# Clustered attention and two MLPs: single refills of operand slots, roots last, normalisation between sums

## The reference

```python
# 1. attention masked by clusters: a query sees the keys of its own cluster alone
scores = np.where(mask, scale * q @ k.T, -1e9)
x = softmax(scores) @ v                      # 1536 tokens x 512
# 2. MLP with a sigmoid gate
h = x @ w_in                                 # 512 -> 2048
x = (h * (1.0 / (1.0 + np.exp(-1.702 * h)))) @ w_out
# 3. MLP with SoLU and a layer norm
h = x @ w_in                                 # 512 -> 1024
sm = np.exp(h - h_max) / (sum(...) + 1e-09)
solu = h * sm
ln = (solu - mu) / np.sqrt(var + 1e-06) * g_ln
out = ln @ w_out                             # 1024 -> 512
```

## Time and profile before

| what | value |
|---|---|
| median of 3 runs | 681.31 us (680.67 to 683.98) |
| the profiled execution | 682.8 us |
| its span, first to last instruction | 681.0 us |
| mean granted clock of TensorE | 0.985 |
| TensorE busy | 636.4 us, 93% |
| VectorE busy | 486.4 us, 71% |
| ScalarE busy | 323.9 us, 48% |
| GpSimd busy | 492.6 us, 72% |

### The profile page before, as it was taken

The page is one execution under the profiler, slowest core; times in us unless marked ns, Lnnn a source line. Parts: engine busy times, 40 slices in busy tenths (PEclk is TensorE's granted clock), DMA queues, the critical chain, the costliest instruction groups (busy, mean ns, idle before and its releaser), DMA issues. The chain is left out here.

```text
span 681.0 us, 11362 instructions
## 1 busy us (share of the span) xinstructions
PE 636.4 (93%) x3245; PEld 531.4 (78%) x3245; DVE 486.4 (71%) x819; ACT 323.9 (48%) x647; POOL 492.6 (72%) x680
## 2 busy tenths in 40 slices
PE   4579999999999999999999999999999987999998
PEld 1269888898989888788877787788888765787876
DVE  3669999999999984757656776674564766677660
ACT  1269999989999884222222222222222422443251
POOL 2567788897888886888888988988886556765400
PEclk9879999999999999999999999999999989999999
DMA  8765553545545421222222222222220000000001
GB/s 283 226 184 142 145 147 97 146 107 146 134 114 136 134 84 63 94 92 92 92 92 92 92 92 92 92 94 92 92 92 0 1 0 16 31 16 17 31 33 46
DMA packets 26936, 64.31 MB, mean 94 GB/s; under 512 B 3872, under 2 KB 10016, under 8 KB 26912
## 3 DMA queue, kind: packets, MB, share of 16 engines
q1 hardware_dynamic: 24896, 60.09, 29.6%
q10 hardware_dynamic: 2016, 3.93, 1.5%
HBM read 46.60 MB, written 4.72 MB: 75 GB/s over the span
## 5 line engine op out<-in xcount | busy, mean ns | idle before, releaser
L1027 DVE TENSOR_TENSOR probs_tl<-banks,probs_th 128x384 fp32r<-128x384 f32 x192 | 100.5, 546 | 11.5 <-ACT probs_th L808 9.0
L1007 DVE TENSOR_REDUCE neg_max<-banks 128x1 f32<-128x768 f32 x96 | 91.1, 949 | 9.6 <-PE banks L530 7.6
L808 ACT CAST probs_th<-banks 128x384 fp32r<-128x384 f32 x192 | 83.2, 485 | 23.7 <-PE banks L543 22.5
L1318 POOL TENSOR_TENSOR wait_scrap<-half_power 128x1 f32<-128x1 f32 x176 | 46.8, 266 | 63.9 <-DVE row_inv L1021 32.1
L797 ACT ACTIVATE probs<-banks,neg_max 128x768 f32<-128x768 f32 x96 | 88.2, 919 | 5.8 <-DVE neg_max L1007 5.8
L1001 DVE TENSOR_TENSOR gl<-gate,gh 128x512 fp32r<-128x512 f32 x48 | 43.8, 912 | 65.1 <-ACT gh L782 65.1
L1394 POOL TENSOR_SCALAR probs<-probs,row_inv 128x768 f32<-128x768 f32 x96 | 87.1, 908 | 0.0
L543 PE MATMUL banks<-ident,probs 128*128 128x128 f32 x576 | 80.1, 275 | 0.6 <-ACT hot_t L751 0.6
L558 PE MATMUL banks<-probs_th,v_parts 128*128 128x384 f32 x192 | 70.4, 367 | 10.0 <-DVE x_sums L1034 10.0
L573 PE MATMUL banks<-xh,uph 128*128 (+1 forms) x192 | 76.7, 400 | 0.9 <-POOL upl L1367 0.7
L782 ACT CAST gh<-gate 128x512 fp32r<-128x512 f32 x48 | 29.8, 620 | 99.8 <-PE banks L590 58.8
(11 more groups left out here) (147 smaller groups left out, 1415.6 us busy)
## 6 DMA issues: line engine op xcount, KB each, us to landing
gelu_raw<-w_gelu SPq DMA_DIRECT2D x48, 512.0 KB, 3.2
ln_raw<-w_ln SPq DMA_DIRECT2D x8, 512.0 KB, 4.8
pair_t<-q_t SPq DMA_DIRECT2D x4, 768.0 KB, 7.7
pair_t<-k_t SPq DMA_DIRECT2D x4, 768.0 KB, 8.9
kq_raw<-k_t SPq DMA_DIRECT2D x16, 192.0 KB, 3.5
kq_raw<-q_t SPq DMA_DIRECT2D x16, 192.0 KB, 3.6
q_parts<-k_high SPq DMA_DIRECT2D x16, 192.0 KB, 2.6
q_high<-k_high SPq DMA_DIRECT2D x16, 192.0 KB, 3.0
```

Of the source, the lines that this page charges most:

```text
L808: nc.scalar.copy(probs_th[half % 2][:, c * CH:(c + 1) * CH, i * P:(i + 1) * P], pt_bank(n, c).rearrange("p (t s) -> p t s", t=CH)).then_in ...
L1007: nc.vector.tensor_reduce(out=neg_max[:, col], in_=scores[n % 2], op=ALU.max, axis=mybir.AxisListType.XY, negate=True).then_inc(max_done, 1)
L1027: nc.vector.tensor_tensor(probs_tl[half % 2][at], pt_bank(n, c).rearrange("p (t s) -> p t s", t=CH), probs_th[half % 2][at].bitcast(F32), ...
```

## The change

- GpSimd no longer waits for all seven products of the pair before. Each split waits for the product that reads its slot, and so does each sum whose target is one of the seven slots.
- lhs_sums and lhs_l get an eighth slot, in which the unsplit sum S4 is kept until its split.
- Both roots stand behind the whole refill.
- VectorE computes both variances of a pair in a row. norm_tile of pair it-1 moves into pair it: u = 0 behind u2_sum, u = 1 behind u3_sum; those of the last pair come at the end.
- In pair 1, lnt_low(0, 0) stands behind c11_sum instead of in front of it.
- The counts on the semaphore stat_step follow the new order.

```diff
--- before.py
+++ after.py
@@ -135,9 +135,9 @@
         rhs_l = sb("rhs_l", [P, 3, KT // 2, BANK], F32R)
         lhs_h = sb("lhs_h", [P, PRODUCTS, KT // 2, P], F32R)
         unsplit_lhs = ExitStack()
-        lhs_sums = sb("lhs_sums", [P, PRODUCTS, KT // 2, P], F32, unsplit_lhs)
+        lhs_sums = sb("lhs_sums", [P, PRODUCTS + 1, KT // 2, P], F32, unsplit_lhs)
         unsplit_lhs.close()
-        lhs_l = sb("lhs_l", [P, PRODUCTS, KT // 2, P], F32R)
+        lhs_l = sb("lhs_l", [P, PRODUCTS + 1, KT // 2, P], F32R)
         raw34.close()
         ln_low = sb("ln_low", [P, UNITS, BANK], F32R, side="right")
         hid = [[hid0[:, v, :] for v in range(2)], [gelu_raw[:, 2 + v, :] for v in range(2)]]
@@ -323,6 +323,8 @@
         def x2_tile(it, row, half):
             at = (2 * it + 1 - row) * P
             return x_sums[:, half * HK:(half + 1) * HK, at:at + P]
+
+        S4_EXACT = PRODUCTS
 
         def lhs_exact(i):
             return lhs_sums[:, i, :, :]
@@ -1179,6 +1181,16 @@
             def st(u, i):
                 return stat[:, u, i:i + 1]
 
+
+            def solu_step(it, u):
+                return it * 8 + u * 2 + 2
+
+            def variance_step(it, u):
+                return it * 8 + 4 + u + 1
+
+            def norm_step(it, u):
+                return it * 8 + 6 + u + 1
+
             def quarter(it, u, c):
                 return hid[it % 2][u][:, c * BANK:(c + 1) * BANK]
 
@@ -1237,7 +1249,7 @@
                 nc.vector.tensor_scalar(st(u, 3), st(u, 2), -1.0 / F2, None, ALU.mult).then_inc(mean_done, 1)
 
                 nc.vector.tensor_scalar(st(u, 5), st(u, 1), 1e-9, None, ALU.add).then_inc(stat_step, 1)
-                dve.wait_ge(stat_step, it * 8 + u * 2 + 1)
+                dve.wait_ge(stat_step, solu_step(it, u) - 1)
                 nc.vector.reciprocal(st(u, 6), st(u, 5)).then_inc(stat_step, 1)
 
             def lnt_low(it, u):
@@ -1250,18 +1262,18 @@
 
             def variance(it, u):
                 dve.wait_ge(square_done, it * 2 + u + 1)
-                dve.wait_ge(stat_step, it * 8 + u * 2 + 2)
+                dve.wait_ge(stat_step, solu_step(it, u))
 
                 nc.vector.tensor_scalar(st(u, 7), st(u, 4), st(u, 6), st(u, 6), ALU.mult, ALU.mult
                                         ).then_inc(stat_step, 1)
-                dve.wait_ge(stat_step, it * 8 + 4 + u * 2 + 1)
+                dve.wait_ge(stat_step, variance_step(it, u))
                 nc.vector.tensor_scalar(st(u, 8), st(u, 7), 1.0 / F2, 1e-6, ALU.mult, ALU.add).then_inc(var_done, 1)
 
             def norm_tile(it, u):
                 t = it * 2 + u
                 dve.wait_ge(root_done, t + 1)
                 nc.vector.reciprocal(st(u, 10), st(u, 9)).then_inc(stat_step, 1)
-                dve.wait_ge(stat_step, it * 8 + 4 + u * 2 + 2)
+                dve.wait_ge(stat_step, norm_step(it, u))
                 nc.vector.tensor_tensor(st(u, 11), st(u, 10), st(u, 6), ALU.mult).then_inc(scale_done, 1)
                 dve.wait_ge(scale_done, t + 1)
                 nc.vector.tensor_scalar(hid[it % 2][u], hid[it % 2][u], st(u, 3), st(u, 11), ALU.add, ALU.mult
@@ -1269,28 +1281,32 @@
 
             for it in range(PAIRS):
                 u2_sum(it)
+                if it >= 1:
+                    norm_tile(it - 1, 0)
                 u4_sum(it)
                 u3_sum(it)
+                if it >= 1:
+                    norm_tile(it - 1, 1)
+                c11_sum(it)
                 if it == 1:
                     lnt_low(0, 0)
-                c11_sum(it)
                 c21_sum(it)
                 c22_sum(it)
                 max_tile(it, 0)
                 c12_sum(it)
                 max_tile(it, 1)
                 solu_tile(it, 0)
+                if it == 1:
+                    lnt_low(0, 1)
                 if it > 1:
                     lnt_low(it - 1, 0)
-                if it == 1:
-                    lnt_low(0, 1)
                 solu_tile(it, 1)
-                variance(it, 0)
-                norm_tile(it, 0)
-                variance(it, 1)
-                norm_tile(it, 1)
+                for u in range(2):
+                    variance(it, u)
                 if it > 1:
                     lnt_low(it - 1, 1)
+            for u in range(2):
+                norm_tile(PAIRS - 1, u)
             for u in range(2):
                 lnt_low(PAIRS - 1, u)
 
@@ -1453,6 +1469,7 @@
 
             def lhs_split(it, order, i, src):
                 first = (it - 1) * LHS_STEPS + order
+                pool.wait_ge(product_done, (it - 1) * PRODUCTS + i + 1)
                 if first > 0:
                     pool.wait_ge(lhs_step, first)
                 nc.gpsimd.tensor_scalar(lhs_h[:, i, :, :], src, 1.0, 1.0, ALU.mult, ALU.mult).then_inc(lhs_step, 1)
@@ -1461,6 +1478,8 @@
                                         ).then_inc(lhs_step, 1)
 
             def lhs_sum(it, order, i, left, right, op):
+                if i < PRODUCTS:
+                    pool.wait_ge(product_done, (it - 1) * PRODUCTS + i + 1)
                 pool.wait_ge(lhs_step, (it - 1) * LHS_STEPS + order)
                 nc.gpsimd.tensor_tensor(lhs_exact(i), left, right, op).then_inc(lhs_step, 1)
 
@@ -1470,20 +1489,19 @@
 
             for it in range(1, PAIRS):
                 pool.wait_ge(x2_done, KT + (it // (BL // (2 * P)) + 1) * KT)
-                pool.wait_ge(product_done, it * PRODUCTS)
                 lhs_split(it, 0, A11, x2_tile(it, 0, 0))
                 lhs_sum(it, 2, S1, x2_tile(it, 1, 0), x2_tile(it, 1, 1), ALU.add)
                 lhs_sum(it, 3, S2, lhs_exact(S1), x2_tile(it, 0, 0), ALU.subtract)
-                lhs_sum(it, 4, S4, x2_tile(it, 0, 1), lhs_exact(S2), ALU.subtract)
+                lhs_sum(it, 4, S4_EXACT, x2_tile(it, 0, 1), lhs_exact(S2), ALU.subtract)
                 lhs_split(it, 5, S2, lhs_exact(S2))
                 lhs_split(it, 7, S1, lhs_exact(S1))
-                root(it - 1, 0)
                 lhs_sum(it, 9, S3, x2_tile(it, 0, 0), x2_tile(it, 1, 0), ALU.subtract)
                 lhs_split(it, 10, S3, lhs_exact(S3))
                 lhs_split(it, 12, A12, x2_tile(it, 0, 1))
                 lhs_split(it, 14, A22, x2_tile(it, 1, 1))
-                lhs_split(it, 16, S4, lhs_exact(S4))
-                root(it - 1, 1)
+                lhs_split(it, 16, S4, lhs_exact(S4_EXACT))
+                for u in range(2):
+                    root(it - 1, u)
             for u in range(2):
                 root(PAIRS - 1, u)
```

## The result

The kernel after took 672.73 us (median of 4 runs, 672.26 to 676.86) against 681.85 us for the kernel before, run beside it (median of 4 runs, 680.67 to 683.98). The ratio is 0.9876, 95% interval 0.983 to 0.9923. The forecast was 675.7 us, in a range from 673.0 to 679.0. The profiled execution took 672.86 us, its span 671.0 us.

The account below looks back on a forecast made before the run. TensorE was taken to bound the last stage from pair 3 on, with the loss in pairs 1 and 2. Gains 6.0 - 0.34 + 0.3 = 6.0 us, less 0.4 for the clock, took 681.31 to 675.7 us; range 673.0 to 679.0.

Parts of the forecast that it names:

- two new waits: TensorE in the last stage: 3.1 us before turn2(0,0) for the norm, about 2 us before turn2(1,1) for lnt_low(1,0).
- Pair 1: Last stage, first product of pair 1 to that of pair 2: ends at 559.07 instead of 562.43, gain 3.4 us.
- The fall: TensorE's clock dropping to 1.2 GHz after the new waits, as likely as not: 0.8 us at pair 3, half counted, 0.4.
- Pair 2: Last stage, up to the start of pair 3: down2(1,0) ends at 584.3 against 590.35, gain in all 6.0 us.
- THREE's forecast wait: In pair 2, TensorE's product THREE waits 0.5 to 0.8 us for u3.
- Pairs 3 and 4: Steady pairs: c21 0.17 us late because the norms stand between VectorE's sums, costing 0.17 us in each pair.
- Pair 5: Tail: lnt_low(4,1) no longer stands behind both norms, so turn2(5,0) need not wait; gain 0.3 us.
- A: Rival: stalls move to turn2(0,0) and turn2(1,1), each followed by a clock fall; gain 3.0 us, 678.3 us; chance 0.17.
- B: Rival: no contention, norms at 1.12 us, and no clock fall; gain 7.3 us, 674.0 us; chance 0.20.
- C: Rival: VectorE bounds the sums, c21 2.5 us late in pairs 2, 3 and 4; loss 1.7 us, 683.0 us; chance 0.05.
- D: Rival: something else holds u2_sum, so only the slot waits are won; gain 2.0 us, 679.3 us; chance 0.08.
- The signs: Trace checks: pair 3 starts at 584.3, then 22.9 to 23.1 us a pair, L1265 near 0.5 us, stage before 539 unmoved.

Follow-up runs that it names:

- norms_only: Kernel after with GpSimd again waiting for all seven products before its refill; no difference from the kernel before that can be told from nothing, pairs 3 and 4 22.50 us.
- after_again: The kernel after, unchanged, run once more beside other kernels; 674.76 us against 682.63 us for the kernel before.
- slots_roots: Kernel after with VectorE's list as before, so norms in their old place, single refills and roots last kept; 2.3 us faster than the kernel after on the stage.
- slots_only: Kernel before with only the single refills and the spare slot, first root still in the middle of the refill; 2.0 us slower on the stage.
- roots_only: Kernel before with only the first root moved behind the whole refill, so both roots are last; 1.0% slower, 7.0 us on the stage.

## Why the prediction was right, and where it was not

*Place and mechanism: right.* Refill at once behind the last split_down, slots in time, second root at 540.30 (536.2 + 4.1; forecast 539.0 + 4.4 to 4.9), two new waits in front of turn2(0,0) and turn2(1,1): all there. The refill itself took 14.9 us and not 13.6; its added waits were priced at nothing, which did no harm because the second root waits for its variance.

*The time: below the range.* 672.73 us is 0.3 us under the range's lower end. The terms below missed by more than their sum did: the gain in pair 1 was forecast 1.4 us too high, that in pair 2 1.7 us too low. That the stage comes within 1.5 us of the forecast is in part luck.

*Pair 1: forecast 3.4 us, measured 2.04.* The wait was 2.69 and not 3.1, but seven matmuls ran at the lower clock, and pair 2 started 1.3 us later against pair 1 than forecast. The fall was priced, but as a half of 0.8 at pair 3.

*Pair 2: forecast 2.6, measured 4.27.* This term was mis-sized most. c21(2) was forecast at 11.0 us behind the pair's first product and came at 567.01 - 557.58 = 9.43. Three things make up these 1.6 us. First, with the fall of the clock pair 2 began 1.3 us later than forecast, but c21(1), which leads to one_copy(2), only 0.5 us later (549.95 - 536.20 = 13.75 behind the first product, forecast 552.25 - 539.01 = 13.24), so that the chain met the pair 0.8 us earlier. Second, one_copy came 560.93 - 549.95 = 10.98 behind c21(1) instead of 11.34; the first product of solu_tile in between, the row at 554.46, took 0.36 us less than at 559.34 in the kernel before:

```profile
559.34 1.70 DVE L1233 CUSTOM_DVE_ANT_0 gelu_raw<-gelu_raw,exp 128x1024 f32<-128x1024 f32 x1
```

```profile
554.46 1.34 DVE L1245 CUSTOM_DVE_ANT_0 gelu_raw<-gelu_raw,exp 128x1024 f32<-128x1024 f32 x1
```

Third, one_copy(2) to c21(2) took 0.4 us less: in pairs 1 and 2 a norm beside GpSimd cost about 0.3 us more than alone, the second of pair 2 nothing, where I had put 0.5. From c21(2) to turn2(1,1) it took 7.7 us, as forecast, and THREE's forecast wait of 0.5 to 0.8 us for u3 did not come.

*Pairs 3 and 4: forecast a loss of 0.17 us each, measured a gain of 0.24 and 0.26.* The step itself was right: c21_sum of pair 3 stands 589.90 - 581.23 = 8.67 behind the start (8.55 forecast). What I left out is that the first product of solu_tile, which stands between c21 and lnt_low, would no longer meet GpSimd in the same way. In the kernel before, in pair 3, with the wait of TensorE that follows:

```profile
603.17 0.74 POOL L1465 TENSOR_TENSOR lhs_sums<-x_sums,lhs_sums 128x256 f32<-128x256 f32 x1
603.24 1.75 DVE L1233 CUSTOM_DVE_ANT_0 gelu_raw<-gelu_raw,exp 128x1024 f32<-128x1024 f32 x1
...
606.71 1.06 PE L700 MATMUL banks<-ident,hid 128*128 128x128 f32 x8 [0.19 <-DVE xh L1247]
```

The 128x1024 product started when GpSimd's sum, with two inputs, had run for 0.07 of its 0.74 us, and took 1.75 us. In the kernel after:

```profile
587.56 0.74 POOL L1484 TENSOR_TENSOR lhs_sums<-x_sums,lhs_sums 128x256 f32<-128x256 f32 x1
...
587.70 0.62 DVE L1277 TENSOR_TENSOR stat<-stat 128x1 f32<-128x1 f32 x1
...
594.07 0.40 POOL L1475 TENSOR_SCALAR lhs_h<-x_sums 128x256 fp32r<-128x256 f32 x1 [0.16 <-POOL lhs_l L1477]
...
594.41 1.22 DVE L1245 CUSTOM_DVE_ANT_0 gelu_raw<-gelu_raw,exp 128x1024 f32<-128x1024 f32 x1
...
594.56 1.68 POOL L1477 TENSOR_TENSOR lhs_l<-x_sums,lhs_h 128x256 fp32r<-128x256 f32 x1
```

Here it started when a split was all but done, and took 1.22; now GpSimd's next operation took 1.68. So c21 comes 0.29 us later against its pair and the product behind it takes 0.53 us less, and TensorE's wait of 0.19 us in front of turn2(2,1) is gone. (The second product of solu_tile got longer, 1.58 us against 1.21; no wait of TensorE followed from it.) The multiply at 587.70 ended as the sum beside it did. In these three rows the engine that starts first runs at full pace and the other gets longer. The Trainium skill, "SBUF — State Buffer", section "🔬 SBUF: two separate sides", has this rule, and these rows agree with it. The instruction that started second got 0.53, 0.46 and 0.94 us longer, where the first still had 0.67, 0.60 and 1.07 us to run. I used the rule for the norms alone and not for what the shifted refill does to VectorE's other operations. That alignment decides is argued from these rows and from the 22.50 us of norms_only, where the first product took 1.22 us as well; no kernel changed the alignment alone, and what separates 22.50 from 22.62 us is not known.

*Pair 5: forecast 0.3, measured 0.37.*

*The sum.* 6.0 us were forecast for the stage before the clock, 5.6 with it, and 7.1 measured. The difference between the medians is 9.1 us, 2 us more. In the set with after_again it is 682.63 - 674.76 = 7.9 us, and the least gain in that set's interval, 1 - 0.9896 = 1.0%, is 7.1 us; so the stage alone can be all of it, but need not be.

*Rivals.* Of A's two falls of the clock one came, and its gain of 3.0 was too small; B, without contention or fall, named 7.3 us and comes nearest in size, but by the wrong mechanism, since both contention and a fall were there. C was refuted: c21 was late by 0.29 us in pair 3, not 2.5. D was refuted: TensorE has no wait for u2_sum left, which in pair 1 starts 6.05 us behind the first product, 11.69 before.

*The signs.* Pair 3 began 45.0 us behind pair 1 (45.3 forecast), and pairs 3 and 4 stayed far under 23.5 us. Some signs failed. Pairs 3 and 4 took 22.6 us and not 22.9 to 23.1. The multiply of norm_tile was to take near 0.5 us in most cases; it did in three of twelve (0.49, 0.62, 0.62) and took 0.16 in the others, while the tile behind it took 1.11 and 1.14 us in front of u4 in pairs 1 and 2. And the stage before 539 did move, by 2.8 us in the first profile and by 1.0 in after_again, which the prediction had named as a sign of being wrong; see "The start" above.

*What the prediction missed in kind.* I priced the norm's new place as a wait in the forecast and still took the whole set of edits as one. Had I asked what the first two edits give without the third, the same rows would have suggested that VectorE, which stood 4.68 us in norm_tile, had room for both norms in their old place; slots_roots shows it.

## What to carry to other kernels

When an engine's list holds both bulk refills and a small step on another engine's critical path, neither starting the refill earlier nor moving the small step helps alone; only the two together did (9.5 us against losses of 2.0 and 7.0). Price each edit of a set without the others, and ask of each moved step what it is put behind: the norm was put behind a sum that waited for a third engine. Where operations of two engines lengthen each other, as VectorE's and GpSimd's do here, a shift of one schedule changes durations elsewhere, so look at every operation that it meets.

## What the runs showed of the hardware

One more wait in front of a GpSimd instruction cost about 0.08 us: the gap between a split's second operation and the next instruction is 0.16 us in the kernel after (the row at 594.07), and 535.20 - 534.38 - 0.74 = 0.08 in the kernel before. The granted clock fell in or behind waits of TensorE of 2.4 us and more (before, after, after_again, slots_only, norms_only, roots_only), and not at all in the stage of the kernels whose waits stayed under 1.5 us. It did not fall each time: not behind the 3.32 us in the earlier trace rows, the 3.1 us of slots_only in pair 1 or the 3.0 us of norms_only in pair 2.
